# Choosing and fetching the first expert item during attention, in a fused attention, expert and feed-forward kernel

## The chip, the cores and the metric

The kernel runs as one program on one core of one Trainium2 chip. The metric is the device time of one execution in microseconds (us); lower is better. The engines are PE (TensorE, matmuls, with its weight loads shown as PEld), DVE (VectorE), ACT (ScalarE), POOL (GpSimd) and SP (SyncE, which here only issues DMAs).

## The reference

Three stages follow one another. All data is fp32.

```python
# 1 attention: q, k, v of shape (4, 12, 448, 64)
q_n, k_n = rmsnorm(q, g_q), rmsnorm(k, g_k)
attn = softmax(q_n @ k_n.T / 8);  x = attn @ v        # then (4*448, 768) tokens
# 2 experts: 8 experts, one per token
logits = normalize(x) @ normalize(expert_emb).T / tau
e = argmax(logits);  gate = softmax(logits)[e]
x = gate * (relu(x @ w1[e]) @ w2[e])                  # w1 768x1024, w2 1024x768
# 3 feed-forward: h = x @ w_in; out = max(0.01 * h, h) @ w_out   # 768x2048, 2048x768
```

## The kernel before

To keep fp32 accuracy every product is made of three matmuls on operands split in two parts: a rounded high part (type fp32r, made by ACT, `w1_hi`) and the rest (`w1_lo` = raw minus high, made by DVE, some of it by POOL).

**Attention** (`attention`, lines 15 to 483) goes over 48 heads (4 batches of 12), software-pipelined: iteration m of every engine's loop works on heads m-2 to m+2 at once, in an order written out by hand per engine. For the next head ACT squares q and k (L311), DVE sums (L394), POOL takes the power -0.5 (L159, L161), splits v (L147), scales and splits k (L177, L183, L187) and scales q (L193); PE transposes them (L229, L236), makes scores (L221, L222), transposes the probabilities (L244), multiplies by v (L258, L259) and by `mix` (L266), which folds the two halves of v's split and appends 8 expert logits of this head. DVE takes the row maxima (L401), splits the probabilities (L407) and stores the scaled result to `x_tok` (L421). POOL's order in an iteration is `split_k`, `norm_q`, `invert_rms`, `split_v`, `norm_k`, `norm_k_hi`, `guard_sums` (lines 197 to 211). SP loads the heads, writes x to `x_rows` in DRAM six heads late (L106), and between them loads the 14 chunks of expert 0's w1 and w2.

**Routing** (`routing`, lines 510 to 788) is a stage of its own behind a barrier of all engines. DVE sums the logits over heads, finds each token's expert (one-hot), counts, ranks within the expert, and makes of rank and expert a slot: an item (128 tokens of one expert, 21 items) and a lane. PE turns the table round (16 matmuls, L626) so that each slot knows its row of x (`slot_rows`). ACT squares x for the norms (L612) and DVE makes the gates.

**Experts** (`experts`, lines 791 to 1149): for item n POOL gathers 128 rows of x (L880), PE transposes them (L933), `product1` (L953 to L955, 6 chunks of 6 matmuls), relu on ACT (L1029), `transpose_h` (L964), `product2` (L983 to L985, 8 chunks of 6 matmuls), and POOL scatters the result (L886). SP loads an item's weights only where the expert is a new one; the split into high and low part is made again for every item. In the steady state `product2` of item n-1 stands between `product1` of items n and n+1, so that PE has work while item n+1 is split:

```python
    product1(n)
    transpose_x(n + 1, 1 - u)
    product2(n - 1, 1 - u, 0, C2 // 2)
    transpose_h(n, u)
    product2(n - 1, 1 - u, C2 // 2, C2)
```

**Feed-forward** (`feed_forward`, line 1152 on) gathers the rows by tiles, scales them by the gates and makes the two products.

The functions that the change touches:

## Time and profile before

| | |
|---|---|
| time, median of 3 runs (lowest, highest) | 1293.85 us (1293.66, 1295.03) |
| profiled execution: own time, its span | 1296.19 us, 1294.5 us |
| busy, share of the span: PE, DVE, ACT, POOL | 95%, 69%, 59%, 43% |
| mean granted clock of TensorE | 0.973 |
| attention, from the start to the last `x_tok` | 0 to 350.3 us |
| routing, then experts, to the last `product2` | 351.6 to 371.8, then to 776 us |
| DMA | 126.4 MB, mean 98 GB/s |

The span is the time from the first to the last instruction of the profiled execution. Its own time is 2.3 us above the median of the runs. An engine's busy share says how long it worked, not whether anything waited for it. A granted clock of 1.00 is 2.4 GHz, of 0.50 1.2 GHz.

### The profile page before, as it was taken

The page shows a single profiled execution, that of the slowest core. Times are in us where ns is not written, and L with a number is a line of the kernel's source. Part 1 is how long each engine was busy: PE and PEld are TensorE (multiplying, and loading weights), DVE is VectorE, ACT ScalarE, POOL GpSimd, SP SyncE. Part 2 cuts the span into 40 slices and gives each one's busy share as a digit, 9 for nine tenths or more (in the row PEclk, how much of TensorE's full clock was granted, in tenths as well). Part 3 has the DMA queues.
Part 4 walks back from the last instruction along what each step waited for, and adds up shares of the span by engine and source line. Part 5 has one row for each costly group of instructions (what it writes and reads, how often), then busy time and mean ns, then how long its engine had stood idle before and what let it go on. Part 6 is the DMA issues. An engine that isn't in the chain of part 4 may idle for free. (4 is left out here: it accounts for less than half of the span.)

```text
span 1294.5 us, 21003 instructions
## 1 busy us (share of the span) xinstructions
PE 1226.4 (95%) x6890; PEld 1097.1 (85%) x6890; DVE 894.2 (69%) x1257; ACT 757.6 (59%) x1434; POOL 553.3 (43%) x581
## 2 busy tenths in 40 slices
PE   5999999999748999999999995999999999999998
PEld 4888888888637988998899884999999999999997
DVE  4999999999757999999999973554432245552222
ACT  4999999999748777877787754222331122221111
POOL 6888888888335777667766740000000000000000
PEclk8999999999959999999999996999999999999999
DMA  1234333322103643664364014112232322211122
GB/s 50 75 103 116 97 105 93 83 67 72 29 28 120 244 142 128 244 244 147 124 242 147 38 49 122 49 49 62 74 92 62 91 65 74 70 44 49 56 86 73
DMA packets 99977, 126.42 MB, mean 98 GB/s; under 512 B 28568, under 2 KB 81048, under 8 KB 99872
## 3 DMA queue, kind: packets, MB, share of 16 engines
q1 hardware_dynamic: 92416, 103.07, 26.0%
q0 software_dynamic: 3360, 16.52, 3.5%
q10 hardware_dynamic: 4096, 5.51, 1.2%
q8 instruction: 57, 0.93, 0.3%
q14 instruction: 48, 0.39, 0.1%
HBM read 193.88 MB, written 19.27 MB: 165 GB/s over the span
## 5 line engine op out<-in xcount | busy, mean ns | idle before, releaser
L1010 ACT CAST w_hi<-w_raw 128x768 fp32r<-128x768 f32 (+1 forms) x294 | 249.7, 931 | 14.5 <-DMA w_raw<-moe_w_in 13.4
L1080 DVE TENSOR_TENSOR w_lo<-w_raw,w_hi 128x1024 fp32r<-128x1024 f32 x84 | 186.9, 2261 | 9.7 <-POOL w_lo L899 7.0
L1490 DVE TENSOR_TENSOR out_lo<-out_raw,out_hi 128x384 fp32r<-128x384 f32 x64 | 35.7, 558 | 169.5 <-ACT out_hi L1399 169.5
L1281 PE MATMUL ps_acc<-yT_hi,in_hi 128*128 128x448 f32 x384 | 142.9, 372 | 2.1 <-DVE yT_lo L1476 2.1
L899 POOL TENSOR_TENSOR w_lo<-w_raw,w_hi 128x1024 fp32r<-128x1024 f32 x42 | 105.8, 2520 | 91.3 <-ACT w_hi L1010 91.0
L1311 PE MATMUL ps_acc<-gT_hi,out_hi 128*128 128x448 f32 x384 | 142.6, 371 | 0.0
L1393 ACT ACTIVATE small_h<-ps_acc 128x448 f32<-128x448 f32 x64 | 34.9, 545 | 183.4 <-PE ps_acc L1283 183.4
L1282 PE MATMUL ps_acc<-yT_hi,in_lo 128*128 128x448 f32 x384 | 141.9, 370 | 0.0
L1283 PE MATMUL ps_acc<-yT_lo,in_hi 128*128 128x448 f32 x384 | 141.9, 369 | 0.0
L1313 PE MATMUL ps_acc<-gT_lo,out_hi 128*128 128x448 f32 x384 | 140.5, 366 | 0.0
L1312 PE MATMUL ps_acc<-gT_hi,out_lo 128*128 128x448 f32 x384 | 140.4, 366 | 0.0
L1399 ACT CAST out_hi<-out_raw 128x384 fp32r<-128x384 f32 x64 | 32.8, 513 | 179.9 <-PE ps_acc L1313 179.6
L1089 DVE TENSOR_TENSOR w_lo<-w_raw,w_hi 128x768 fp32r<-128x768 f32 x126 | 135.1, 1137 | 0.0
L407 DVE TENSOR_TENSOR pT_lo<-ps_pt,pT_hi 112x448 fp32r<-112x448 f32 x192 | 115.1, 620 | 27.6 <-ACT pT_hi L355 27.5
L346 ACT ACTIVATE probs<-ps_s,neg_max 112x448 f32<-112x448 f32 x192 | 122.7, 644 | 3.6 <-DVE neg_max L401 3.6
L1498 DVE TENSOR_TENSOR g_sb<-ps_acc,small_h 128x448 f32<-128x448 f32 x64 | 40.0, 625 | 116.3 <-ACT small_h L1393 116.3
L983 PE MATMUL ps_y<-w_hi,hT_hi 128*128 128x384 f32 x336 | 116.8, 348 | 1.5 <-issue 1.3
L893 POOL TENSOR_TENSOR w_lo<-w_raw,w_hi 128x768 fp32r<-128x768 f32 x42 | 105.7, 2518 | 22.9 <-ACT w_hi L1010 21.4
L401 DVE TENSOR_REDUCE neg_max<-ps_s 112x1 f32<-112x448 f32 x192 | 113.3, 610 | 2.0 <-PE ps_s L222 1.8
L984 PE MATMUL ps_y<-w_lo,hT_hi 128*128 128x384 f32 x336 | 113.5, 338 | 0.0
L985 PE MATMUL ps_y<-w_hi,hT_lo 128*128 128x384 f32 x336 | 113.5, 338 | 0.0
L953 PE MATMUL ps_h<-w_hi,xT_hi 128*128 128x512 f32 x252 | 101.3, 402 | 4.8 <-DVE w_lo L1080 2.9
(182 smaller groups left out, 2999.7 us busy)
## 6 DMA issues: line engine op xcount, KB each, us to landing
w_raw<-moe_w_in SPq DMA_DIRECT2D x84, 1536.0 KB
in_raw<-moe_w_in_in SPq DMA_DIRECT2D x32, 384.0 KB, 3.3
out_raw<-moe_w_out_in SPq DMA_DIRECT2D x64, 192.0 KB, 2.4
qk_raw<-q_in SPq DMA_DIRECT2D x48, 112.0 KB, 2.1
qk_raw<-k_in SPq DMA_DIRECT2D x48, 112.0 KB, 2.2
v_raw<-v_in SPq DMA_DIRECT2D x48, 112.0 KB, 2.0
x_rows<-x_tok SPq DMA_DIRECT2D x48, 112.0 KB, 2.5
out_rows<-o_sb ACTq DMA_DIRECT2D x26, 168.0 KB, 2.4
```

The costliest lines, as they stand in the source:

```text
L346: act.activation(probs[:, t, :], ps_s[0:R, t, 0:S], ACT.Exp, bias=neg_max[u][:, t:t + 1], accum_out=sums[u][:, t:t + 1]).then_inc(s_exp, 1)
L407: dve.tensor_tensor(pT_lo[u][:, :, cols], src, pT_hi[u][:, :, cols].bitcast(F32), ALU.subtract).then_inc(s_plo, 1)
L983: pe.matmul(out, hT_hi[u][:, c, :], w2_hi[:, c, cols], start=c == 0, stop=False)
L1010: act.copy(out[:, c, :], raw[:, c, :]).then_inc(s_hi, 1)
L1080: dve.tensor_tensor(w1_lo[:, c, :], w1_raw[:, c, :], w1_hi[:, c, :].bitcast(F32), ALU.subtract).then_inc(s_w1lo, 1)
L1089: dve.tensor_tensor(w2_lo[:, c, :], w2_raw[:, c, :], w2_hi[:, c, :].bitcast(F32), ALU.subtract).then_inc(s_w2lo, 1)
L1281: pe.matmul(h, in_hi[u][:, c, :], yT_hi[:, c, cols], start=c == 0, stop=False)
L1282: pe.matmul(h, in_lo[u][:, c, :], yT_hi[:, c, cols], start=False, stop=False)
L1283: last = pe.matmul(h, in_hi[u][:, c, :], yT_lo[:, c, cols], start=False, stop=c == C - 1)
L1311: pe.matmul(acc, out_hi[u][:, lhs], hi, start=first, stop=False)
L1312: pe.matmul(acc, out_lo[u][:, lhs], hi, start=False, stop=False)
L1313: last = pe.matmul(acc, out_hi[u][:, lhs], lo, start=False, stop=final)
```

## The change

The routing stage goes as a stage. What of it concerns the first three batches is done in attention, the rest at the head of the expert stage:

- POOL adds each head's 8 logits to a running sum (`add_logits`, in every iteration from 2 on), makes the index tables in iterations 4 to 7 (`tables`), the lane one-hots of the 12 early tiles in iterations 42 and 43 (`early_lanes`) and the gather of the first item's rows in iteration 45.
- DVE chooses the experts of three batches at the end of iteration 38, counts in 40, places in 41 and takes the expert with the most tokens as the first (`item_expert[0]`), turns the expert order in 42; PE has `early_ranks` (2 matmuls) and `first_rows` (12) before two of its `outputs`. SP loads the chosen expert's w1 and w2 behind the loads of heads 46 and 47.
- The first item's x is transposed and split at the end of attention (`transpose_first`, `x_hi_first`, `x_lo_first`).
- The expert stage begins with the last batch's choice on DVE, while ACT splits w1 high and POOL makes three chunks of `w1_lo`; PE's `place` (the table turned round) stands in the middle of `product1(0)`. Items 0 and 1 are of one expert and use one split; `product2(0)` is made before `product1(1)`.
- The squares of x for the gates are made from `x_rows`, one tile per item on ACT, and the gates at item 19 and 20.
- The rows of `x_rows` and `y_rows` are in the order of the output. `mix` holds 12 heads instead of 48, and the expert embeddings lie in `w1_raw`.

```diff
-    x_dest = x_rows.rearrange("(p t b) d -> p t (b d)", t=T, b=B)
+    x_dest = x_rows.rearrange("(b p t) d -> b p t d", p=R, t=T)
...
-        mix = sb("mix", [P, N, X])
+        mix = sb("mix", [P, H, X])
...
-                sp.dma_start(x_dest[:, :, bass.ds(n * D, D)], x_tok[:, :, bass.ds(n, 1), 0:D].rearrange("p t o d -> p t (o d)")).then_inc(s_x_out, 16)
+                sp.dma_start(x_dest[n // H, :, :, n % H * D:(n % H + 1) * D], x_tok[:, :, n, 0:D]).then_inc(
+                    s_x_early if n < EARLY else s_x_out, 16)
...
+            def first_weights(e, w, raw, C, s_in):
+                src = w[bass.ds(e, 1), :, :].rearrange("o (c p) n -> p (o c) n", p=P)
+                for k in range(2):
+                    chunks = slice(k * C // 2, (k + 1) * C // 2)
+                    sp.dma_start(raw[:, chunks, :], src[:, chunks, :]).then_inc(s_in[k], 16)
...
+                if n == N - 2:
+                    sp.wait_ge(s_pick, 1)
+                    e = sp.value_load(rt["item_expert"][0:1, 0:1], min_val=0, max_val=E - 1)
+                    first_weights(e, w1, w1_raw, C1, s_w1_in)
+                if n == N - 1:
+                    first_weights(e, w2, w2_raw, C2, s_w2_in)
...
+            def add_logits(n):
+
+                part = x_tok[:, :, n, D:X]
+                total = logits[:, n // H * T:(n // H + 1) * T, :]
+                pool.wait_ge(s_xc, n + 1)
+                if n % H == 0:
+                    pool.tensor_copy(total, part).then_inc(s_lg, 1)
+                else:
+                    pool.wait_ge(s_lg, n)
+                    pool.tensor_tensor(total, total, part, ALU.add).then_inc(s_lg, 1)
+            def early_lanes(m):
+
+                if m in (EARLY + 6, EARLY + 7):
+                    pool.wait_ge(s_lane, 1)
+                    pool.wait_ge(s_tables, 6)
+                    half = m - EARLY - 6
+                    for j in range(half * J0 // 2, (half + 1) * J0 // 2):
+                        last = pool.tensor_scalar(in_lane[:, j, :], rt["lane_index"][:, :], lane_f[:, j:j + 1], rt["row_plus"][:, j:j + 1],
+                                                  ALU.is_equal, ALU.mult)
+                    last.then_inc(s_in_lane, 1)
+                if m == EARLY + 9:
+                    pool.wait_ge(s_row_first, 1)
+                    pool.wait_ge(s_x_early, 16 * EARLY)
...
+                tables(m)
+                if m >= 2:
+                    add_logits(m - 2)
+                early_lanes(m)
+            add_logits(N - 2)
...
+                if n == EARLY + 2:
+                    early_ranks()
+                if n == EARLY + 7:
+                    first_rows()
...
+            def early_ranks():
+
+                pe.wait_ge(s_hot, 1)
+                some = hot[:, 0:J0, :].rearrange("p j e -> p (j e)")
+                pe.matmul(ps_tot, rt["ones"][:, :], some, start=True, stop=True)
+                pe.matmul(ps_rank, rt["before"][:, :], some, start=True, stop=True).then_inc(s_rank, 1)
+            def first_rows():
+
+                pe.wait_ge(s_in_lane, 2)
+                pe.wait_ge(s_in_first, 1)
+                for j in range(J0):
+                    last = pe.matmul(ps_row, in_lane[:, j, :], in_first[:, j, :], start=j == 0, stop=j == J0 - 1)
+                last.then_inc(s_first, 1)
+            def transpose_first():
+
+                pe.wait_ge(s_x_first, 16)
+                pe.wait_ge(s_exp, (N - 1) * T + 2)
+                for c in range(C1):
+                    last = pe.transpose(ps_s[:, c // 3, (c % 3) * P:(c % 3 + 1) * P], x_first[:, c * P:(c + 1) * P], ident[:, :])
+                last.then_inc(s_xt, 1)
...
+                if m == N - 1:
+                    transpose_first()
                 if m - 1 >= 0:
                     outputs(m - 1, (m - 1) % 2)
...
+                if n == EARLY + 2:
+                    early_totals()
+                if n == EARLY + 7:
+                    rows_of_first()
...
+            def early_choice():
+
+                dve.memset(scan[0][:, 0:8, :], 0.0).then_inc(s_step, 1)
+                dve.memset(scan[1][:, 0:8, :], 0.0).then_inc(s_step, 1)
+                dve.tensor_reduce(top[:, 0:J0], some, AX.X, ALU.max).then_inc(s_step, 1)
+                dve.tensor_tensor(is_top[:, :, :], some, top[:, 0:J0].unsqueeze(2).to_broadcast([R, J0, E]), ALU.is_equal).then_inc(s_step, 1)
+                dve.tensor_tensor(cand[:, :, :], is_top[:, :, :], e_index[:, :, :], ALU.mult).then_inc(s_step, 1)
+                dve.tensor_reduce(first_top[:, 0:J0], cand[:, :, :], AX.X, ALU.min).then_inc(s_step, 1)
+                dve.tensor_tensor(hot[:, 0:J0, :], e_index[:, :, :], first_top[:, 0:J0].unsqueeze(2).to_broadcast([R, J0, E]),
+                                  ALU.is_equal).then_inc(s_hot, 1)
+            def early_counts():
+                for k, hop in enumerate((1, 2, 4, 8)):
+                    a, b = scan[k % 2], scan[1 - k % 2]
+                    dve.tensor_tensor(b[:, 8:8 + J0, :], a[:, 8:8 + J0, :], a[:, 8 - hop:8 + J0 - hop, :], ALU.add).then_inc(s_step, 1)
+                dve.tensor_copy(rt["counts"][:, :], scan[0][:, 8 + J0 - 1, :]).then_inc(s_step, 1)
+                dve.tensor_tensor(ranks[:, :, :], ranks[:, :, :], scan[0][:, 8:8 + J0, :], ALU.add).then_inc(s_step, 1)
+                dve.tensor_tensor(ranks[:, :, :], ranks[:, :, :], hot[:, 0:J0, :].bitcast(F32), ALU.mult).then_inc(s_step, 1)
+                dve.tensor_reduce(rank_f[:, :], ranks[:, :, :], AX.X, ALU.add).then_inc(s_step, 1)
+            def early_places():
+                dve.tensor_copy(rank_i[:, :], rank_f[:, :]).then_inc(s_step, 1)
+                dve.tensor_scalar(lane_i[:, :], rank_i[:, :], P - 1, None, ALU.bitwise_and).then_inc(s_step, 1)
+                dve.tensor_scalar(blk_i[:, :], rank_i[:, :], 7, None, ALU.logical_shift_right).then_inc(s_step, 1)
+                dve.tensor_copy(blk_f[:, 0:J0], blk_i[:, :]).then_inc(s_step, 1)
+                dve.tensor_copy(lane_f[:, 0:J0], lane_i[:, :]).then_inc(s_lane, 1)
+                dve.tensor_reduce(most[:, :], rt["counts"][:, :], AX.X, ALU.max).then_inc(s_step, 1)
+                dve.scalar_tensor_tensor(most_e[:, :], rt["counts"][:, :], most[:, 0:1], e_index[:, 0, :], ALU.is_equal, ALU.mult).then_inc(s_step, 1)
+                dve.tensor_reduce(rt["chosen"][:, :], most_e[:, :], AX.X, ALU.min).then_inc(s_step, 1)
+                dve.tensor_scalar(rt["item_expert"][:, 0:1], rt["chosen"][0:1, :], float(E), None, ALU.add).then_inc(s_pick, 1)
+            def early_turn():
+                dve.tensor_scalar(turned[:, :], e_index[:, 0, :], rt["chosen"][:, 0:1], None, ALU.subtract).then_inc(s_step, 1)
+                dve.tensor_scalar(wrapped[:, :], turned[:, :], 0.0, float(E), ALU.is_lt, ALU.mult).then_inc(s_step, 1)
+                dve.tensor_tensor(turned[:, :], turned[:, :], wrapped[:, :], ALU.add).then_inc(s_step, 1)
+                dve.tensor_tensor(rt["ahead"][:, :, :], turned[:, :].unsqueeze(2).to_broadcast([R, E, E]),
+                                  turned[:, :].unsqueeze(1).to_broadcast([R, E, E]), ALU.is_gt).then_inc(s_step, 1)
+                dve.tensor_scalar(hit[:, :], first_top[:, 0:J0], rt["chosen"][:, 0:1], None, ALU.is_equal).then_inc(s_step, 1)
+                dve.wait_ge(s_step, 28)
+                dve.scalar_tensor_tensor(in_first[:, :, :], blk_f[:, 0:J0].unsqueeze(2).to_broadcast([R, J0, 2]), 0.0,
+                                         hit[:, :].unsqueeze(2).to_broadcast([R, J0, 2]), ALU.is_equal, ALU.mult).then_inc(s_in_first, 1)
+            def rows_of_first():
+
+                dve.wait_ge(s_first, 1)
+                dve.tensor_scalar(row_first[:, :], ps_row[:, 0:1], -1.0, None, ALU.add).then_inc(s_row_first, 1)
...
+            def last_logits():
+                total = logits[:, J0:J, :]
+                dve.tensor_tensor(total, total, x_tok[:, :, N - 1, D:X], ALU.add).then_inc(s_step, 1)
...
+                if m == EARLY + 2:
+                    early_choice()
+                if m == EARLY + 4:
+                    early_counts()
+                if m == EARLY + 5:
+                    early_places()
+                if m == EARLY + 6:
+                    early_turn()
+                if m == N:
+                    x_lo_first()
+            last_logits()
...
+    def splits(i):
+
+        return max(i - 1, 0)
+    def pool1(s):
+        return (0, 1, 2) if s == 0 else (1, 4)
+
+    def pool2(s):
+        return (1, 4, 6) if s == 0 else (1, 5)
...
-            load1(0)
-            load1(1)
-            load2(0)
-            for i in range(items - 2):
-                load1(i + 2)
+            load1(2)
+            for i in range(2, items):
+                if i + 1 < items:
+                    load1(i + 1)
+                load2(i)
+                if 2 <= i - 2 < J:
...
+            def lo1(i):
+                for c in pool1(splits(i)):
...
+            lo1(0)
             gather(1, 1)
-            for c in POOL1:
-                lo1(0, c)
+            gather(2, 0)
+            lo2(0)
...
+                if n >= 3:
+                    lo2(n - 1)
...
+                if n == items - 2:
+                    pool.wait_ge(s_xss, J)
+                    pool.tensor_tensor(x_norm[:, :], x_ss[:, :], consts["half"][0:R, 0:J], ALU.pow).then_inc(s_xnorm, 1)
...
+            def rank():
+                pe.wait_ge(s_hot, 1)
+                late = hot[:, J0:J, :]
+                pe.matmul(ps_tot, rt["ones"][:, :], late.rearrange("p j e -> p (j e)"), start=True, stop=True).then_inc(s_tot, 1)
+                pe.matmul(ps_rank, rt["before"][:, :], late.rearrange("p j e -> p (j e)"), start=True, stop=False)
+                for j in range(T):
+                    last = pe.matmul(ps_rank[:, j * E:T * E], rt["ones"][:, :], late[:, j:j + 1, :].to_broadcast([R, T - j, E]),
+                                     start=False, stop=j == T - 1)
+                last.then_inc(s_rank, 1)
+            def place():
+                pe.wait_ge(s_place, 1)
+                for j in range(J):
+                    if j >= J0:
+                        pe.wait_ge(s_place, j - J0 + 2)
+                    last = pe.matmul(ps_slot, in_lane[:, j, :], in_item[:, j, :], start=j == 0, stop=j == J - 1)
+                last.then_inc(s_put, 1)
...
-            transpose_x(0, 0)
+            rank()
+            product1(0, 0, C1 // 2)
+            place()
+            product1(0, C1 // 2, C1)
+            transpose_h(0, 0)
+            transpose_x(1, 1)
+            product2(0, 0, 0, C2)
...
+            def square_x(j):
+                act.wait_ge(s_chk[j % 2], uses(j, j % 2))
+                act.activation(x_chk[j % 2], x_chk[j % 2], ACT.Square, accum_out=x_ss[:, j:j + 1]).then_inc(s_xss, 1)
...
+                if 0 <= n - FIRST_CHK < J:
+                    square_x(n - FIRST_CHK)
...
+            for semaphore, count in stored:
+                act.wait_ge(semaphore, count)
+            for c in range(C2):
+                hi2(0, c)
+            relu(0, 0)
+            relu(0, 1)
+            h_hi(0, 0)
+            x_hi(1)
...
-            slot_column(0, 0)
+            late_choice()
+            block_starts()
+            late_places()
+            item_places()
+            rows_of_slots()
             slot_column(1, 1)
+            slot_column(2, 0)
             for c in range(C1):
-                if c not in POOL1:
-                    lo1(0, c)
-                if c == 2:
-                    x_lo(0)
+                lo1(0, c)
+            experts_of_items()
+            for c in range(C2 // 2):
+                lo2(0, c)
+            h_lo(0, 0)
+            x_lo(1)
+            for c in range(C2 // 2, C2):
+                lo2(0, c)
...
+                if n == items - 2:
+                    gate_exponents()
...
+            gates()
...
```

On POOL, in a head of the second batch. Before (L153 is `guard_sums`, L187 `split_k`):

```order
L177 TENSOR_TENSOR k_n<-qk_raw,rstd 112x256
L183 TENSOR_TENSOR k_hl<-qk_raw,rstd 112x4x64
L153 TENSOR_TENSOR sums_eps<-sums,eps_sum 112x4
L187 TENSOR_TENSOR k_hl<-k_n,k_hl 112x4x64
L193 TENSOR_TENSOR q_n<-qk_raw,rstd 112x4x64 x2
```

and now (L187 is `guard_sums`, L221 `split_k`):

```order
L211 TENSOR_TENSOR k_n<-qk_raw,rstd 112x256
L217 TENSOR_TENSOR k_hl<-qk_raw,rstd 112x4x64
L187 TENSOR_TENSOR sums_eps<-sums,eps_sum 112x4
L264 TENSOR_TENSOR logits<-logits,x_tok 112x32
L221 TENSOR_TENSOR k_hl<-k_n,k_hl 112x4x64
L227 TENSOR_TENSOR q_n<-qk_raw,rstd 112x4x64 x2
```

The addition of the logits has come between the two.

On DVE, at the end of attention's iteration 38. Before, the maxima of the next head (L401) are followed by the splits of this one (L407) and `x_tok`:

```order
L411 SCALAR_TENSOR_TENSOR qT_lo<-ps_tr,gain,qT_hi 128x448
L407 TENSOR_TENSOR pT_lo<-ps_pt,pT_hi 112x4x112
L401 TENSOR_REDUCE neg_max<-ps_s 112x1 x2
L407 TENSOR_TENSOR pT_lo<-ps_pt,pT_hi 112x4x112 x2
L421 TENSOR_TENSOR x_tok<-ps_ux,inv_sums 112x4x72
L401 TENSOR_REDUCE neg_max<-ps_s 112x1
```

and now, the seven instructions L590 to L602 of `early_choice` between L527 (maxima) and L533 (splits):

```order
L527 TENSOR_REDUCE neg_max<-ps_s 112x1 x2
L590 MEMSET scan 112x64
L591 MEMSET scan 112x64
L594 TENSOR_REDUCE top<-logits 112x12
L596 TENSOR_TENSOR is_top<-logits,top 112x96
L598 TENSOR_TENSOR cand<-is_top,e_index 112x96
L600 TENSOR_REDUCE first_top<-cand 112x12
L602 TENSOR_TENSOR hot<-e_index,first_top 112x96
L533 TENSOR_TENSOR pT_lo<-ps_pt,pT_hi 112x4x112 x2
L551 TENSOR_TENSOR x_tok<-ps_ux,inv_sums 112x4x72
```

`early_counts`, `early_places` and `early_turn` stand at the same place two, three and four iterations later.

On PE, at the head of the expert stage. Before:

```order
L933 MATMUL ps_xm<-ident,x_g 128x128 x6
L953 MATMUL ps_h<-w_hi,xT_hi 128x512
L954 MATMUL ps_h<-w_lo,xT_hi 128x512
L955 MATMUL ps_h<-w_hi,xT_lo 128x512
L953 MATMUL ps_h<-w_hi,xT_hi 128x512
L954 MATMUL ps_h<-w_lo,xT_hi 128x512
```

and now (L954 to L957 rank the last batch, L966 is `place`; 18 matmuls of `product1(0)` stand on either side of it):

```order
L954 MATMUL ps_y<-hot,ones 112x32
L955 MATMUL ps_y<-hot,before 112x32
L994 MATMUL ps_h<-w_hi,xT_hi 128x512
L995 MATMUL ps_h<-w_lo,xT_hi 128x512
L996 MATMUL ps_h<-w_hi,xT_lo 128x512
...
L966 MATMUL ps_y<-in_item,in_lane 128x22 x16
L994 MATMUL ps_h<-w_hi,xT_hi 128x512
L995 MATMUL ps_h<-w_lo,xT_hi 128x512
L996 MATMUL ps_h<-w_hi,xT_lo 128x512
```

The transposes of item 0 are gone from here, and the placing has come in.

## Rows read from the trace of the kernel before

**Rows 1.** Four stretches by engine: us, busy time (instructions), PE clock, DMA share, GB/s.

```profile
100.00:200.00 100.00, 99.66 (x715) 86.12 (x714) 91.48 (x178) 97.56 (x253) 84.96 (x134) 1.00 0.37 100
360.00:370.00 10.00, 3.63 (x16) 3.49 (x16) 8.65 (x31) 4.92 (x12) 3.32 (x1) 0.50 0.00 0
430.00:440.00 10.00, 10.00 (x56) 9.19 (x55) 10.00 (x10) 7.34 (x9) 6.67 (x3) 1.00 0.99 386
500.00:600.00 100.00, 100.00 (x542) 91.47 (x541) 100.00 (x83) 79.15 (x100) 68.27 (x32) 1.00 0.54 199
```

**Rows 2.** Timeline of one attention head: start, duration, engine, line, out<-in [idle before<-releaser].

```profile
251.25 1.15 DVE L407 TENSOR_TENSOR pT_lo<-ps_pt,pT_hi 112x448 fp32r<-112x448 f32 x2
251.36 0.73 POOL L187 TENSOR_TENSOR k_hl<-k_n,k_hl 112x256 fp32r<-112x256 f32 x1
252.03 0.17 PEld L222 LDWEIGHTS ps_s<-kT,qT_lo 128*112 128x112 f32 x1
252.23 0.53 PEld L229 LDWEIGHTS ps_tr<-ident,k_hl 112*128 112x128 f32 x4
254.12 0.20 POOL L159 TENSOR_TENSOR meansq<-sumsq,eps_d 112x8 f32<-112x8 f32 x1 [0.88 <-DVE sumsq L394]
255.50 0.41 ACT L323 CAST v_hl<-v_raw 112x256 fp32r<-112x256 f32 x1 [0.17 <-PE ps_ux L259]
255.99 0.73 POOL L147 TENSOR_TENSOR v_hl<-v_raw,v_hl 112x256 fp32r<-112x256 f32 x1
257.95 0.20 POOL L153 TENSOR_TENSOR sums_eps<-sums,eps_sum 112x4 f32<-112x4 f32 x1
```

**Rows 3.** Timeline of ACT: one copy per head, 41 heads apart.

```profile
61.63 0.53 ACT L317 COPY u_sb<-ps_ux 128x448 f32<-128x448 f32 x1
...
337.69 0.53 ACT L317 COPY u_sb<-ps_ux 128x448 f32<-128x448 f32 x1
```

**Rows 4.** Timeline: last store of attention, then relu of items 0, 1, 2 and 20.

```profile
349.88 0.46 DVE L421 TENSOR_TENSOR x_tok<-ps_ux,inv_sums 112x288 f32<-112x288 f32 x1 [3.53 <-PE ps_ux L266]
...
391.70 1.09 ACT L1029 ACTIVATE h_sb<-ps_h 128x512 f32<-128x512 f32 x2 [9.25 <-PE ps_h L955]
407.30 1.09 ACT L1029 ACTIVATE h_sb<-ps_h 128x512 f32<-128x512 f32 x2 [1.38 <-PE ps_h L955]
426.10 1.09 ACT L1029 ACTIVATE h_sb<-ps_h 128x512 f32<-128x512 f32 x2 [2.85 <-PE ps_h L955]
...
756.68 1.09 ACT L1029 ACTIVATE h_sb<-ps_h 128x512 f32<-128x512 f32 x2 [2.86 <-PE ps_h L955]
```

**Rows 5.** Timeline near the start of attention.

```profile
8.30 1.77 DVE L434 COPY mix<-fold 128x3072 f32<-128x3072 f32 x1
8.53 2.00 POOL L177 TENSOR_TENSOR k_n<-qk_raw,rstd 112x256 f32<-112x256 f32 x1
```

**Rows 6.** Timeline of POOL in routing: first and last of 11 table instructions.

```profile
351.57 0.19 POOL L586 MEMSET not_before<- 112x112 f32 x1 [7.44 <-POOLq L31]
...
353.48 0.15 POOL L602 IOTA free_row<- 128x21 f32 x1
```

**Rows 7.** Timeline of routing and the first gather.

```profile
354.89 0.29 DVE L646 TENSOR_TENSOR is_top<-logits,top 112x128 f32<-112x128 f32 x1
...
361.52 0.17 DVE L712 CAST slot_i<-slot_f 112x16 int32<-112x16 f32 x1
364.42 3.63 PE L626 MATMUL ps_slot<-in_item,in_lane 112*128 112x66 f32 x16 [6.95 <-DVE in_lane L733]
372.93 1.21 POOL L880 DMA_INDIRECT x_g<-x_rows,slot_in  x1 [4.61 <-DVE slot_in L1071]
```

**Rows 8.** Timeline in the expert stage: a DVE split beside POOL's, and one alone.

```profile
503.34 2.39 POOL L899 TENSOR_TENSOR w_lo<-w_raw,w_hi 128x1024 fp32r<-128x1024 f32 x1 [1.98 <-ACT w_hi L1010]
503.92 2.89 DVE L1080 TENSOR_TENSOR w_lo<-w_raw,w_hi 128x1024 fp32r<-128x1024 f32 x1
...
394.45 1.23 DVE L1080 TENSOR_TENSOR w_lo<-w_raw,w_hi 128x1024 fp32r<-128x1024 f32 x1
```

790 lines of the change are left out of this document (392 added, 398 removed).

## The prediction

> **What bounds the kernel now.** I read first the busy times of four stretches, to see which engine has room in which stage [rows 1]. In attention (the first row) PE works 99.7 of 100 us, ACT 97.6, DVE 91.5 and POOL 85: nothing is free there. In routing (the second) PE works 3.6 of 10 us, with a granted clock of 0.50, while DVE is busy with small operations. In the steady experts (the last) PE works all the time at clock 1.00, and item follows item without a gap; ACT works 79% of it.
>
> Then the timeline of one head [rows 2], to see who waits for whom at its shortest margin. `split_k` on POOL ends at 251.36 + 0.73 = 252.09, and PE loads it at 252.23 (L229): with about 0.06 for the semaphore, 0.08 us of slack. POOL's chain cannot start earlier, since `split_v` waits for ACT's rounding of v (255.50 + 0.41, then 255.99). On DVE the split L407 follows with no idle time before it, so what is put ahead of it comes late nearly whole. A head takes (337.69 - 61.63) / 41 = 6.73 us [rows 3].
>
> Last the way from attention to the first products [rows 4]: attention ends at 350.3, the routing stage starts at 351.6, the first relu of item 0 stands at 391.7 and that of item 2 at 426.1, 74.5 us behind 351.6. Of these, 41 us lie ahead of the first relu, and this is what the change attacks. From item 2 on, item follows item at (756.68 - 426.10) / 18 = 18.37 us, with ACT idle for 2.86 before each relu.
>
> The profiled execution took 1296.2 us itself, 2.3 above the median of 1293.85. I make the sum against 1296.2 and take 2.3 off at the end.
>
> **Attention, part by part.**
> A. `mix` is a quarter as large. Its copy took 1.77 us and a `k_n` beside it 2.00 [rows 5]. Gain 1.3 (bounds 0 and 2).
> B. `add_logits`, 46 times on POOL between `guard_sums` and `split_k`. Nothing in the trace has 224 elements; the nearest are 0.20 us for 4 and for 8 elements a partition and 0.73 for 256 [rows 2], which gives 0.20 + 28 x 2.1 ns = 0.26, about 0.20 of it as pitch. Less the 0.08 of slack, `transpose_k` comes 0.12 late in each head: 46 x 0.12 = +5.5. Bounds: 0 if PE or ACT can reorder their waits around it, +9 if nothing is absorbed.
> C. The tables took POOL 353.63 - 351.57 = 2.1 us [rows 6], and stand now in four heads: +2.1 (0 to 2.1).
> D. The early choice on DVE. A 96-element operation costs about 0.28 (0.29 for 128), a tiny one 0.17 to 0.21 [rows 7]. Choice 5 x 0.28 and two memsets, 1.7; totals 0.5; counts 2.2; places 9 x 0.2 = 1.8: +6.2. The turn, 1.3, lies beside POOL's lanes, which are longer. DVE operations also queue behind a running POOL operation: a 1024-element split took 2.89 beside POOL's and 1.23 alone [rows 8]. A POOL operation of attention takes 84.96 / 134 = 0.63 us and one runs 85% of the time [rows 1], so an operation that queues waits 0.85 x 0.32 = 0.27. Of the 21 or so here I take this for 6, those that read two SBUF tiles as the split does: +1.5 (0 to 5.5).
> E. Lane one-hots, 12 on POOL, 112 elements each in two heads. Between 0.20 and 0.73 [rows 2] I take 0.33 by the elements: +4.0 (3 to 5.5).
> F. PE: 14 matmuls, 0.23 each at half clock [rows 7], so about 0.12 at the full one: +1.7.
> G. The gather holds POOL 1.21 [rows 7] ahead of `transpose_k`: +1.3.
> H. Six more transposes at the end and the last heads' loads behind 3.1 MB of w1, which take 8 us at 386 GB/s [rows 1] where the loads have about a head and a half of lead: +0.8 (0 to 4).
> Sum: -1.3 + 5.5 + 2.1 + 6.2 + 1.5 + 4.0 + 1.7 + 1.3 + 0.8 = **+21.8**, bounds +12 and +29. Attention should end at about 372.
>
> **The start of the experts,** counted from the barrier. Both weights should be there: 6.3 MB take 16 us at 386 GB/s and are issued two and one heads before the end. POOL makes three chunks of `w1_lo` (2.4 to 2.8 each), until 9.1. Meanwhile DVE does the late choice, about 28 small operations up to the last batch's lanes, at the pitch of [rows 7]; I let three queue behind POOL's long ones. That leaves some 14 of them behind 9.1, and puts these lanes at 9.1 + 14 x 0.25 = 12.7, the slots, rows and two columns, which wait for the 16 matmuls of `place` (3.6 at half clock, [rows 7]), at 16.2; then DVE's three chunks of `w1_lo`, 1.23 each [rows 8], to 19.9. PE, which stood with clock 0.50 as in the second row of [rows 1], does the last chunk behind them, in all about 4 more by half clock for the first chunk and full for the rest. The first relu comes at 24.0. From there to the relu of item 1: the relu pair 1.1 [rows 4], eight transposes 0.9, rounding 1.1, split 1.2 with semaphores make 4.5, and then `product2(0)` and `product1(1)`, which together are an item less its 14 transposes, 18.4 - 1.6 = 16.8. From relu 1 to 2 nothing stands between but `product1`, as between 0 and 1 before: 407.30 - 391.70 = 15.6 [rows 4]. Item 2's relu stands at 24.0 + 21.3 + 15.6 = 60.9, against 74.5: **-13.6**. With the first relu at 18.5 (no queueing) it is -19, at 28 (POOL and DVE in series) -9.6. From item 2 on the order of products is the old one.
>
> **The end.** The gates, four DVE operations and POOL's power behind item 20, stand now before the feed-forward's first tiles: +0.6 (0 to 3). `square_x`, about 0.9 + 0.2 per item on ACT (a relu pair of 1024 elements takes 1.09), fits into its 2.86 of idle time: 0. If ACT's cover were gone it would cost 16 x 1 us.
>
> Net: 21.8 - 13.6 + 0.6 = **+8.8**: 1305.0 by this execution, 1302.6 by the median. In short, routing loses its 20 us of its own, but its operations come back where every engine is full, and the first item's cold start stays.
>
> **Rivals.**
> 1. Faster: idle times in a head take up the small work. For it speaks that POOL stands 0.88 idle before L159 and ACT 0.17 before L323 [rows 2], and DVE works only 91.5% [rows 1], 0.6 us a head. Then `add_logits`, tables and the queueing cost nothing (B, C, the 1.5 of D), and of the other inserts (6.2 + 4.0 + 1.7 + 1.3 + 0.8 = 14.0) a quarter vanishes. Attention -1.3 + 10.5 = +9.2, net 9.2 - 13.6 + 0.6 = -3.8: 1290.1. Against it: the idle time lies before L159, and the short margin before L229; POOL cannot work ahead of ACT's v. It decides by one point: whether L229 starts later. Chance 0.32.
> 2. All small operations queue. In the trace only large ones do, 2.89 beside 2.39 [rows 8], and 2.00 for the `k_n` of 256 elements beside a DVE copy [rows 5]. If the other 15 of D wait 0.27 each too, attention gets 4 more. Of the late choice only one operation then runs at each seam between POOL's, some 24 instead of 14 are left behind 9.1, and with their pitch of 0.25 the first relu comes 3 later: 8.8 + 7 = 15.8, 1309.6. Chance 0.18.
> The Trainium skill, SBUF — State Buffer, "Who interferes with whom", says that DVE and GpSimd share one pair of ports, which an instruction locks until it ends, and that this holds for a DVE instruction with two SBUF inputs or in a two-port mode. By that rule, the trace agrees for the large ones: DVE's split ends about when POOL's and then its own time have passed [rows 8]. It would put plain fp32 copies between SBUF tiles into the queue too, and by it the time is that of this rival; no row of before shows a small one blocked.
> 3. None of the small operations queues: -1.5 in D and the first relu at 18.5, -5.5 in the start. Net 8.8 - 1.5 - 5.5 = +1.8: 1295.7. Chance 0.12.
> 4. The change does not do what it says: the first weights or rows are late. At the 199 GB/s of the last row of [rows 1] the 6.3 MB need 32 us, where some 12 to 25 are to be had before the barrier. w1, which goes first, needs 16 of them; the gathered rows beside it then come 2 us late, and w2 is wanted only 20 us behind the barrier: +2, 1304.6. Chance 0.04.
>
> **How the numbers follow.** My forecast, 1302.6 with 1297 to 1309 as its own range, has 0.34. About 0.2%, 2.6 us, is what a measurement of this kernel can tell from no change, so 1291.3 to 1296.4 is the same. Faster takes rival 1 for the most part (0.29) and 0.03 of rival 3; same takes 0.03 of rival 1, 0.07 of rival 3 and 0.05 from the forecast's and rival 4's low end; the rest, 0.53, is slower. The range must reach from rival 1 with half of its own width below, 1285, to rival 2 with as much above, 1315.
>
> **What would show it.** In the profile of after: ACT's head period at 6.85 instead of 6.73 with L229's counterpart waiting for POOL's `split_k` (B); heads 38 to 45 longer by 12 to 15 us together (D to G); the last `x_tok` near 372; DVE's small operations no longer than 0.3 except beside POOL's splits (rivals 2 and 3); PE idle with clock 0.50 in the first 10 us of the experts; the first relu 24 and item 2's 61 us behind the barrier. I am wrong if the head period stays 6.73, which makes rival 1 the case; if the first relu comes beyond 28, which adds its delay whole; or if PE waits between items 2 and 20, where I cost everything at nothing.

## The result and the profile after

The changed kernel takes 1314.17 us (median of 4 runs, 1311.04 to 1319.03) against 1294.28 for the kernel before on the same chip: a ratio of 1.0157 with an interval of 1.0120 to 1.0194, 19.9 us slower. The forecast was 8.8 slower, the range reached to 1315. A second set of four runs gave 1312.19 and 1.0149 (1.0132 to 1.0167). The profiled execution took 1319.03 itself, span 1317.3, so it shows 22.8 us more than the span before, some 3 to 5 more than the medians do.

| stretch of the profiled execution | before | after | difference | forecast |
|---|---|---|---|---|
| attention, to the end of the last `x_tok` | 350.3 | 377.0 | +26.7 | +21.8 |
| from the next stage's start to item 2's relu | 74.5 | 62.5 | -12.0 | -13.6 |
| relu 2 to relu 20 | 330.6 | 332.8 | +2.2 | 0 |
| relu 20 to the feed-forward's first transpose | 30.9 | 38.0 | +7.1 | +0.6 |
| from there to the end of the span | 506.9 | 505.7 | -1.2 | 0 |

The stage's start is POOL's first table before, 351.6, and ACT's first rounding of w1 after, 378.3; both lie 1.2 us behind attention.

Stretches of after by engine (us; busy time and instructions of PE, PEld, DVE, ACT, POOL; PE clock, DMA share, GB/s), as in [rows 1]:

```profile
100.00:200.00 100.00, 99.71 (x714) 84.94 (x713) 91.14 (x179) 97.46 (x254) 88.39 (x150) 1.00 0.27 70
323.00:325.00 2.00, 0.00 (x0) 0.00 (x0) 2.00 (x6) 0.00 (x0) 2.00 (x3) 1.00 0.00 0
327.00:329.00 2.00, 2.00 (x10) 1.96 (x10) 0.00 (x0) 1.20 (x4) 1.92 (x4) 0.50 0.05 8
380.00:384.00 4.00, 2.84 (x10) 2.39 (x10) 3.93 (x3) 4.00 (x6) 4.00 (x2) 0.50 0.61 172
```

Attention in its middle is as full as it was. New are the second and third row: PE did nothing for 2 us in the middle of attention, and then ran with a granted clock of 0.50. The fourth row is the head of the experts.

ACT's copy of each head, as in [rows 3]:

```profile
136.54 0.53 ACT L436 COPY u_sb<-ps_ux 128x448 f32<-128x448 f32 x1
...
284.94 0.53 ACT L436 COPY u_sb<-ps_ux 128x448 f32<-128x448 f32 x1
...
334.13 0.54 ACT L436 COPY u_sb<-ps_ux 128x448 f32<-128x448 f32 x1
...
347.94 0.53 ACT L436 COPY u_sb<-ps_ux 128x448 f32<-128x448 f32 x1
...
364.19 0.53 ACT L436 COPY u_sb<-ps_ux 128x448 f32<-128x448 f32 x1
```

The first two copies are 22 heads apart: where only `add_logits` is inserted a head takes 6.745 us, against 6.735 before. The head before 334.13 took 14.4 and the next 13.8. Over heads 38 to 45, from 284.94 to 364.19, the trace has 25.4 us more than eight times 6.735, over heads 4 to 14 (the tables) 2.2.

What `add_logits` (L264) does in a head, as in [rows 2]:

```profile
252.43 0.25 POOL L264 TENSOR_TENSOR logits<-logits,x_tok 112x32 f32<-112x32 f32 x1
252.65 0.74 POOL L221 TENSOR_TENSOR k_hl<-k_n,k_hl 112x256 fp32r<-112x256 f32 x1
253.43 0.41 PEld L320 LDWEIGHTS ps_tr<-ident,k_hl 112*128 112x128 f32 x4 [0.16 <-POOL k_hl L221]
253.50 0.55 PE L320 MATMUL ps_tr<-ident,k_hl 112*128 112x112 f32 x4
255.73 0.68 ACT L456 ACTIVATE qT_hi<-ps_tr,gain 128x448 fp32r<-128x448 f32 x1
```

and before, beside [rows 2], ACT's copy of this head, the k transposes and the rounding of q:

```profile
250.13 0.53 ACT L317 COPY u_sb<-ps_ux 128x448 f32<-128x448 f32 x1
252.43 0.55 PE L229 MATMUL ps_tr<-ident,k_hl 112*128 112x112 f32 x4
254.65 0.68 ACT L337 ACTIVATE qT_hi<-ps_tr,gain 128x448 fp32r<-128x448 f32 x1
```

`split_k` (L221) now ends 2.18 behind the head's copy on ACT (251.21), and PE's weight load waits for it, 0.16. In [rows 2] the same load came 2.10 behind the copy (250.13), now it comes at 2.22: the 0.12 of the forecast. But the load stood 0.20 ahead of its matmul, and this lead takes the delay: the matmuls start 2.29 behind the copy, 2.30 before, and ACT rounds q 4.52 behind it in both. Over ten heads of each trace the medians say the same: load 2.09 before and 2.25 now, matmul 2.29 and 2.30. The delay ends on PE itself.

The head of iteration 42, with POOL's six lane one-hots:

```profile
321.31 4.69 POOL L273 TENSOR_SCALAR in_lane<-lane_index,lane_f,row_plus 112x128 fp32r<-112x128 f32 x6
326.75 1.01 PE L320 MATMUL ps_tr<-ident,k_hl 112*128 112x112 f32 x4 [4.61 <-POOL k_hl L221]
327.80 0.53 ACT L448 CAST kT<-ps_tr 128x448 fp32r<-128x448 f32 x1 [4.92 <-PE ps_tr L320]
```

One one-hot of 128 elements with two scalars from memory takes 4.69 / 6 = 0.78 us on POOL, more than the 0.73 of a subtraction of 256 elements [rows 2]. PE stands 4.61, and its four transposes then take 1.01 instead of 0.55. The clock stands at 0.50 for about 6.8 us in each of the two heads with the one-hots, and for about 3.4 in the one with the counts.

DVE in iterations 38 and 40: the operations that read two SBUF tiles while POOL works,

```profile
286.44 0.72 DVE L596 TENSOR_TENSOR is_top<-logits,top 112x96 f32<-112x96 f32 x1
287.19 0.55 DVE L598 TENSOR_TENSOR cand<-is_top,e_index 112x96 f32<-112x96 f32 x1
...
301.64 1.85 DVE L616 TENSOR_TENSOR scan<-scan 112x96 f32<-112x96 f32 x4
```

0.72, 0.55 and 4 x 0.46 instead of 0.25 to 0.29.

The head of the experts, POOL and DVE, then PE's `place` (L966) and DVE's chunks of `w1_lo`:

```profile
379.42 7.03 POOL L916 TENSOR_TENSOR w_lo<-w_raw,w_hi 128x1024 fp32r<-128x1024 f32 x3 [6.10 <-ACT w_hi L1057]
380.10 1.70 DVE L1148 SCALAR_TENSOR_TENSOR block_i<-totals,counts 112x8 int32<-112x8 f32 x1
381.83 2.31 DVE L1150 TENSOR_SCALAR block_i<-block_i 112x8 int32<-112x8 int32 x1
384.18 2.31 DVE L1152 CAST blocks<-block_i 112x8 f32<-112x8 int32 x1
386.52 0.22 DVE L1154 TENSOR_TENSOR passed<-ahead,blocks 112x64 f32<-112x64 f32 x1
...
389.64 2.36 PE L966 MATMUL ps_y<-in_item,in_lane 112*128 112x22 f32 x16 [0.71 <-DVE in_item L1184]
...
392.60 3.49 DVE L1248 TENSOR_TENSOR w_lo<-w_raw,w_hi 128x1024 fp32r<-128x1024 f32 x3
```

The three chunks of `w1_lo` on POOL take 7.03 us. Beside them an operation of 8 elements takes 1.70, the next two 2.31 each, though the last two read a single tile; the first one that starts when POOL is done takes 0.22. `place` ends at 392.0, 13.7 behind the start, and only then come DVE's chunks 3 to 5.

Behind them an operation of one partition meets POOL's splits of w2, and PE stands 3.83 before `product2(0)` for the low part of h, which stands behind it on DVE:

```profile
396.92 5.43 DVE L1209 TENSOR_SCALAR item_e<-item_e,chosen 1x21 f32<-1x21 f32 x1
...
406.88 0.41 PE L1024 MATMUL ps_y<-w_hi,hT_hi 128*128 128x384 f32 x1 [3.83 <-DVE hT_lo L1268]
```

The relu of items 0, 1, 2 and 20, as in [rows 4]:

```profile
400.16 1.09 ACT L1075 ACTIVATE h_sb<-ps_h 128x512 f32<-128x512 f32 x2 [10.21 <-PE ps_h L996]
...
425.25 1.08 ACT L1075 ACTIVATE h_sb<-ps_h 128x512 f32<-128x512 f32 x2 [21.10 <-PE ps_h L996]
...
440.77 1.09 ACT L1075 ACTIVATE h_sb<-ps_h 128x512 f32<-128x512 f32 x2 [7.14 <-PE ps_h L996]
...
773.56 1.08 ACT L1075 ACTIVATE h_sb<-ps_h 128x512 f32<-128x512 f32 x2 [2.63 <-PE ps_h L996]
```

Item 0's relu stands 21.9 behind the start, item 1's 25.1 behind that, item 2's 15.5 behind that.

The end of the experts: POOL's power, the first of the gates' operations on DVE, the exponent on ACT, and PE's idle time:

```profile
766.55 3.93 POOL L941 TENSOR_TENSOR x_norm<-x_ss,half 112x16 f32<-112x16 f32 x1
770.52 1.82 DVE L1221 TENSOR_SCALAR x_norm<-x_norm 112x16 f32<-112x16 f32 x1
774.60 0.31 ACT L1102 ACTIVATE exps<-shifted 112x128 f32<-112x128 f32 x1
776.51 0.47 PE L1024 MATMUL ps_y<-w_hi,hT_hi 128*128 128x384 f32 x1 [2.99 <-DVE w_lo L1256]
...
811.56 1.35 PE L1446 MATMUL ps_trf<-ident,y_g 112*128 112x112 f32 x6 [11.64 <-ACT y_g L1553]
```

The power holds POOL 3.93 us, DVE's next operation waits for POOL's splits again (1.82 for 16 elements), the exponent and with it ACT's next roundings wait for both, and PE stands 2.99 before `product2(19)`. Yet PE later stands 11.64 before L1446, where the gates could have been made for nothing.

### The profile page after: what moved, and what is told of

It is laid out like the page before. It is cut to its first block and busy times, and to the rows that moved or that the text cites. A ratio compares the mean times of both kernels' runs of the same rounds, so it can differ in the third digit from the quotient of the medians.

```text
span 1317.3 us, 21043 instructions
## 1 busy us (share of the span) xinstructions
PE 1237.8 (94%) x6906; PEld 1101.8 (84%) x6906; DVE 891.9 (68%) x1267; ACT 748.0 (57%) x1420; POOL 558.2 (42%) x638
## 3 DMA queue, kind: packets, MB, share of 16 engines
q1 hardware_dynamic: 94304, 108.58, 26.7%
## 5 line engine op out<-in xcount | busy, mean ns | idle before, releaser
L1057 ACT CAST w_hi<-w_raw 128x768 fp32r<-128x768 f32 (+1 forms) x280 | 238.8, 931 | 22.3 <-DMA w_raw<-moe_w_in 13.4
L1248 DVE TENSOR_TENSOR w_lo<-w_raw,w_hi 128x1024 fp32r<-128x1024 f32 x79 | 173.5, 2232 | 1.7 <-ACT w_hi L1057 1.6
L533 DVE TENSOR_TENSOR pT_lo<-ps_pt,pT_hi 112x448 fp32r<-112x448 f32 x192 | 115.1, 620 | 42.1 <-ACT pT_hi L474 41.9
L1256 DVE TENSOR_TENSOR w_lo<-w_raw,w_hi 128x768 fp32r<-128x768 f32 x119 | 132.3, 1174 | 1.2 <-ACT w_hi L1057 1.2
L527 DVE TENSOR_REDUCE neg_max<-ps_s 112x1 f32<-112x448 f32 x192 | 113.2, 610 | 2.1 <-PE ps_s L313 1.8
L994 PE MATMUL ps_h<-w_hi,xT_hi 128*128 128x512 f32 x252 | 101.5, 403 | 12.1 <-DVE w_lo L1248 10.2
L335 PE MATMUL ps_pt<-ident,probs 112*112 112x112 f32 x768 | 101.1, 265 | 7.1 <-DVE pT_lo L533 7.0
```

What stands on the lines that cost most here:

```text
L1057: act.copy(out[:, c, :], raw[:, c, :]).then_inc(s_hi, 1)
L1248: dve.tensor_tensor(w1_lo[:, c, :], w1_raw[:, c, :], w1_hi[:, c, :].bitcast(F32), ALU.subtract).then_inc(s_w1lo, 1)
L1256: dve.tensor_tensor(w2_lo[:, c, :], w2_raw[:, c, :], w2_hi[:, c, :].bitcast(F32), ALU.subtract).then_inc(s_w2lo, 1)
```

## The experiments

What each kernel shows by stage, from its profiled execution (att: what attention took; 4-14 and 38-45: us over the period of 6.735 in these heads; relu 0: from the stage's start; relu 1: from relu 0; 2-20: relu 2 to 20; end: relu 20 to the feed-forward). The sets a, b and c ran on three chips, on which the kernel before took 1293.97, 1294.88 and 1295.25 us in the median, so that a difference of a microsecond or two between sets says nothing:

| kernel | time, us | att | 4-14 | 38-45 | relu 0 | relu 1 | 2-20 | end |
|---|---|---|---|---|---|---|---|---|
| before | 1294.3 | 350.3 | 0 | 0 | 40.1 | 15.6 | 330.6 | 30.9 |
| changed, first set | 1314.2 | 377.0 | 2.2 | 25.4 | 21.9 | 25.1 | 332.8 | 38.0 |
| a0_again | 1312.2 | 377.0 | 2.3 | 26.3 | 21.3 | 25.4 | 325.7 | 37.8 |
| a1_lanes_dve | 1308.0 | 371.3 | 2.3 | 19.3 | 21.2 | 25.5 | 325.8 | 38.1 |
| a2_gates_end | 1305.5 | 374.9 | 2.2 | 25.4 | 21.9 | 25.1 | 327.5 | 30.7 |
| a3_start | 1311.8 | 375.6 | 2.3 | 23.5 | 15.5 | 27.9 | 329.0 | 37.8 |
| b1_start2 | 1308.6 | 377.3 | 2.3 | 25.4 | 15.1 | 21.6 | 327.4 | 37.2 |
| b2_spread | 1297.0 | 359.6 | 1.9 | 10.2 | 22.5 | 24.2 | 329.9 | 38.7 |
| b3_warm | 1311.0 | 370.6 | 2.6 | 19.0 | 21.1 | 25.6 | 327.6 | 36.6 |
| b4_all | 1280.9 | 361.9 | 2.0 | 9.8 | 15.4 | 21.4 | 329.8 | 30.9 |
| c1_all_again | 1279.5 | 359.1 | 1.9 | 9.9 | 15.4 | 21.6 | 325.7 | 30.7 |
| c2_two_adds | 1324.2 | 384.8 | 4.0 | 27.2 | 21.2 | 25.4 | 332.1 | 38.0 |
| c3_add_behind_q | 1282.2 | 357.6 | 0.2 | 9.3 | 15.1 | 23.1 | 325.9 | 30.8 |

**The changed kernel again.**

> The changed kernel once more, for a second trace and more times. If the delays of attention are fixed ones, the heads take the same times as in the first trace (14.4 and 13.8 us for the two with the lane one-hots on POOL, 10.8 for the one with the counts). The 8 us between its runs (1311 to 1319) I expect in the expert items, where some take 19.9 us and others 18.05: if it comes from there, another number of items is long this time. Time 1311 to 1319.

Attention repeats (377.0; 26.3 over in heads 38 to 45). Within it heads differ by up to 0.9: the one with the counts takes 11.7 for 10.8, the next 9.0 for 8.4, the first with one-hots 13.9 for 14.4. For the first of these the granted clock goes along: it stands at 0.50 for about 6.1 us here and 3.4 in the first trace. Relu 2 to 20 takes 325.7 instead of 332.8: in the first trace items 5, 7 and 9 took 19.9, here none does. That is 7 us, as much as the runs of this kernel scatter, and the place is the expected one. Why some items are long in one execution and not in the next stays open; in these three PE waits 1.2 us for a `w_lo` of DVE.

**The lane one-hots on DVE.** In POOL's iterations 42 and 43 the six operations go, and DVE makes them behind its own at the same iterations:

```diff
-                        last = pool.tensor_scalar(in_lane[:, j, :], rt["lane_index"][:, :], lane_f[:, j:j + 1], rt["row_plus"][:, j:j + 1],
+                        last = dve.tensor_scalar(in_lane[:, j, :], rt["lane_index"][:, :], lane_f[:, j:j + 1], rt["row_plus"][:, j:j + 1],
```

> The 12 early lane one-hots move from POOL to DVE, six at the end of iteration 42 and six in 43. Theory A (they cost 0.78 us each on POOL and stop the chain split_k, transposes, scores; on DVE 0.28 each): the two heads take 6.74 + 1.7 + 1.4 (the turn) and 6.74 + 1.7 instead of 14.4 and 13.8, so 11 us less, about 1303. Theory B (the two heads are long because the first expert's weights load beside them, not because of POOL): the two heads stay over 12 us, and the time falls by less than 4.

```profile
323.31 1.62 DVE L656 TENSOR_SCALAR in_lane<-lane_index,lane_f,row_plus 112x128 fp32r<-112x128 f32 x6
...
332.77 2.79 DVE L656 TENSOR_SCALAR in_lane<-lane_index,lane_f,row_plus 112x128 fp32r<-112x128 f32 x6
```

0.27 each for the first six. The two heads take 11.8 and 10.5 instead of 13.9 and 13.7 in a0_again, 5.4 less; the time falls by 4.2. The one-hots' place is part of the cost, but 11 was too much: DVE's six operations, behind six others, make their head 5.1 longer for 3.9 of work, and the second six take 2.79, queued behind POOL. PE now stands 2.75 and 1.75 in these heads, and its clock falls to 0.50 in both again. Theory B falls: SP issues the first expert's w1 at 335.95 in the first trace, behind the first of the two long heads, and in that head's gap nothing loads (the second of the rows by engine, 0 GB/s).

**The gates at the end.** POOL's power stands behind `store_y` of item 19, the exponent behind ACT's last rounding, DVE's gates behind its last split:

```diff
-                if n == items - 2:
-                    gate_exponents()
...
             for c in range(C2 // 2, C2):
                 lo2(items - 1, c)
+            gate_exponents()
+            gates()
```

> The power on POOL, the exponent on ACT and the gates on DVE stand behind the last splits instead of in items 19 and 20, where PE later stands idle 11.6 us anyway. Theory A (POOL's power of 3.9 us holds up its splits and DVE, and exp on ACT waits for them): from the relu of item 20 to the first transpose of the feed-forward 31 us as before the change instead of 38, time about 6 less, 1308. Theory B (the end is long for another reason, the loads or the order of the last scatters): 38 stays, and the time with it.

```profile
766.16 1.09 ACT L1074 ACTIVATE h_sb<-ps_h 128x512 f32<-128x512 f32 x2 [2.64 <-PE ps_h L995]
...
796.89 1.35 PE L1444 MATMUL ps_trf<-ident,y_g 112*128 112x112 f32 x6 [11.67 <-ACT y_g L1551]
```

30.7 instead of 38.0 from item 20's relu to the feed-forward, 7 us; the medians differ by 6.7. Theory A holds: the end is as short as before the change. Power, exponent and gates moved together, so their shares are not separated.

**DVE alone at the start.** POOL's three chunks of the first `w1_lo` go to DVE, which makes one behind each step of the choice:

```diff
-        return (0, 1, 2) if s == 0 else (1, 4)
+        return () if s == 0 else (1, 4)
...
             late_choice()
+            lo1(0, 0)
             block_starts()
+            lo1(0, 1)
             late_places()
+            lo1(0, 2)
             item_places()
+            lo1(0, 3)
+            lo1(0, 4)
```

> POOL makes no chunk of the first w1_lo; DVE makes all six, one after each step of the late choice; the experts of the items are found before w2 is split. Theory A (three small DVE operations waited 1.7, 2.3 and 2.3 us for POOL's splits, and PE stood 4 us for that): relu of item 0 at 18 us from the start of the stage instead of 22, and item 1's 23 behind it instead of 25; 4 to 6 us less, about 1309. Theory B (what bounds the start is PE at half clock and its own products, not DVE): item 0's relu stays at 21 or later.

DVE (L1150 and L1152 are the two that took 2.31; L1148, which took 1.70, takes 0.17 too), then the last two lines of the search for the items' experts, POOL's `w2_lo` and PE's `product2(0)`:

```profile
379.53 0.17 DVE L1150 TENSOR_SCALAR block_i<-block_i 112x8 int32<-112x8 int32 x1
379.74 0.17 DVE L1152 CAST blocks<-block_i 112x8 f32<-112x8 int32 x1
...
391.82 5.92 DVE L1215 CAST item_expert<-item_e 1x21 int32<-1x21 f32 x1
392.36 5.35 POOL L923 TENSOR_TENSOR w_lo<-w_raw,w_hi 128x768 fp32r<-128x768 f32 x3
...
401.66 0.66 PE L1024 MATMUL ps_y<-w_hi,hT_hi 128*128 128x384 f32 x1 [6.36 <-DVE hT_lo L1268]
```

With POOL idle the three take 0.17 each, and relu 0 comes at 15.5, 6.4 earlier and better than the 18 I expected, at the same clock of 0.50 for PE's first chunks. So the half clock of the first chunks did not bound the start, DVE's wait did. It also brought a second stretch at half clock: in the first trace PE's last three chunks start at 393.96, have the clock at 0.50 until 397.5 and take 6.2, here they start at 388.03 with 1.00 and take 4.4, 1.8 of the 6.4. (The chunks changed engine and place together; of the two, only the queueing is seen in the rows.) But 2.8 come back where I expected a gain of 2: a cast of 21 elements on a single partition takes 5.92, until the last of POOL's three splits, which follow one another without a gap, and PE stands 6.36 for the low part of h behind it. The cast is recorded as starting 0.54 before the first split, so that it met the splits running is not shown. The median falls by 0.4.

**The same without POOL's `w2_lo`.**

```diff
-        return (1, 4, 6) if s == 0 else (1, 5)
+        return () if s == 0 else (1, 5)
```

> As a3_start, and POOL makes none of the first w2_lo either. In a3 a cast of 21 elements on DVE took 5.92 us, as long as POOL's three splits of w2, and PE stood 6.4 us for the low part of h behind it. Theory A (each small DVE operation that meets a running POOL split waits for its end, and for those that follow at once): item 0's relu at 15.5 us from the first rounding of w1 as in a3, item 1's 21.5 behind it instead of 27.9 (25.1 before), together 10 us less than the changed kernel, about 1302. Theory B (PE's half clock and the splits of w2 by DVE alone, eight at 0.9, bound it): item 1's stays over 25 behind.

15.1 and 21.6, item 2's relu at 52.2 instead of 62.2: the 10 us are there to the digit. In the medians only 3.6 show, and the runs of this kernel scatter by 11 us (1304.3 to 1315.3); the stage, of one trace, is what this verdict rests on.

**Early work in three places of a head.** Tables one operation a head over heads 4 to 14; DVE's 42 early operations, lane one-hots among them, from one list, 1 or 2 before each of the splits `split_lo(m, 0)` and `split_lo(m, 1)`, which wait for ACT, and the rest at the end:

```diff
+                    slot(m, 'A')
                     split_lo(m, m % 2, 0)
...
+                    slot(m, 'B')
                     split_lo(m, m % 2, 1)
...
-                if m == EARLY + 2:
-                    early_choice()
+                slot(m, 'C')
```

> In attention: POOL's tables one operation a head over 11 heads; all early work of DVE, the 12 lane one-hots too, in three places of each head (one or two operations before each of the two splits that wait for ACT, the rest at the end) over heads 37 to 44. Theory A (a POOL operation of 0.2 us more per head stays hidden by ACT's squares; small DVE work is free before the splits that wait for ACT, 0.55 us a head; and no stall of PE is long enough to halve its clock): heads 4 to 14 at 6.75, heads 38 to 45 together 12 us over the period instead of 25, time about 14 less, 1298. Theory B (all of it is paid wherever it stands): heads 4 to 14 pay 2.4 us together as before, heads 38 to 45 over 18.

Heads 38 to 45 pay 10.2 instead of 25.4 (and 26.3): theory A, by more than expected. Two things are in this: the one-hots' move to DVE alone had brought 19.3 (a1), the rest is the spreading. Of the four heads with five or six operations two cost 0.8 and 1.3, two 0.2 each; what is left is 4.6 in the one with ten, and 1.5 and 1.3 in the last two, with the other eight one-hots and PE's rows. In the one with ten the clock stands at 0.50 for about 6.4 us; the same head takes 10.6 and 10.7 in b4_all and c1_all_again, with about 3.4 at 0.50, and 9.1 in c3_add_behind_q, where the clock stays 1.00. The tables pay 1.9 instead of 2.3: there theory B holds, an operation of 0.2 on POOL costs 0.17 a head once `add_logits` stands before it. The time falls by 15 to 17.

**Keeping the clock.**

```diff
             def transpose_k(n, u):
-                pe.wait_ge(s_khl, n + 1)
                 if n > 0:
                     pe.wait_ge(s_qlo, n)
+                if n in (EARLY + 8, EARLY + 9):
+                    for i in range(32):
+                        t = i % T
+                        pe.transpose(ps_tr[:, t * R:(t + 1) * R], ident[0:R, :], ident[0:R, 0:R])
+                pe.wait_ge(s_khl, n + 1)
```

> The changed kernel with the lane one-hots on POOL as they were, and 32 transposes of a constant on PE, written where the k transposes go, while PE waits for POOL in the two heads of the one-hots. Theory A (the two heads lose 7.4 us for 4.7 of POOL's work since the granted clock falls to 0.50 after 4 us of idle PE, and the rest of the head runs at half speed): the clock stays 1.00, the heads take 11.7 and 11.4 us instead of 14.2 and 13.8, time 4 to 5 less, about 1308. Theory B (the rest is POOL's own chain for q behind the one-hots): the heads stay as long, or longer by what the extra transposes cost.

POOL's one-hots, the added transposes and the k transposes that follow, then the stretch behind 325.51:

```profile
320.08 4.68 POOL L273 TENSOR_SCALAR in_lane<-lane_index,lane_f,row_plus 112x128 fp32r<-112x128 f32 x6
320.73 3.23 PE L321 MATMUL ps_tr<-ident 112*128 112x112 f32 x32
325.51 0.60 PE L324 MATMUL ps_tr<-ident,k_hl 112*128 112x112 f32 x4 [1.56 <-POOL k_hl L221]
```

```profile
326.00:328.00 2.00, 2.00 (x17) 1.87 (x15) 0.24 (x1) 1.84 (x5) 1.92 (x4) 1.00 0.14 39
```

POOL holds PE as long as before, 4.68, but the transposes take 0.60 instead of 1.01, the clock stays 1.00, and the two heads take 11.6 and 11.4 instead of 13.9 and 13.7, 4.7 less together, as theory A has it. Of the 14.8 us that the first trace shows for the two heads, 5 or so are the clock. (Attention is 6.4 shorter in all; 2.2 of it is the head with the counts, 9.4 here and 11.7 in a0_again, which the edit does not touch: here its clock stays 1.00 too. The same head takes 10.7 to 11.0 in the six traces where it stands at 0.50 for about 3.4 us. Why it did not fall here, no run shows.) The median shows 1.2 of it.

**All in one,** b1, b2 and a2 together, and once more.

> b1_start2, b2_spread and a2_gates_end in one. If the costs lie in three separate stages, they add: 10 + 14 + 7 less than the changed kernel's 1312, about 1281, which is below the kernel before. If they hide one another (the saved time of one stage comes back as a wait for weights in the next), it stays above 1290.

> b4_all once more, with more rounds, for its interval against the kernel before. If its 1280.9 us stands, 1277 to 1287 and a ratio under 0.995; if the first one was a lucky chip or run, above 1290.

The relu of item 2 of c1_all_again, whose first rounding of w1 stands at 360.36:

```profile
412.89 1.09 ACT L1091 ACTIVATE h_sb<-ps_h 128x512 f32<-128x512 f32 x2 [7.12 <-PE ps_h L1012]
```

1280.93, then 1279.51 with a ratio to the kernel before of 0.9875 (0.9854 to 0.9896). The stages add, and this version is 15.7 us faster than the kernel before, 33 faster than the change as made. Attention 359.1 (+8.8), item 2's relu at 52.5 (-22.0), the end 30.7.

**A second addition.** In every head, behind the first, with its result unused:

```diff
                     pool.tensor_tensor(total, total, part, ALU.add).then_inc(s_lg, 1)
+                pool.wait_ge(s_twice, n)
+                pool.tensor_tensor(unused[:, :, :], part, part, ALU.add).then_inc(s_twice, 1)
```

> The changed kernel with a second addition of the same size on POOL in every head, its result unused. The first cost 0.01 us a head although the k transposes came 0.12 later; the tables, one a head on top of it, cost 0.16 each. Theory A (behind the 0.08 us before the transposes lie some 0.15 more, in which ACT is still at its squares, and the first addition has used them up): the second is paid nearly whole, heads at 6.90 to 6.95 us, 7 to 9 us over the whole. Theory B (small POOL work is hidden by its 0.7 us of idle time in each head, and the tables cost something else): the heads stay at 6.75.

```profile
202.64 0.23 POOL L268 TENSOR_TENSOR unused<-x_tok 112x32 f32<-112x32 f32 x1
202.83 0.74 POOL L223 TENSOR_TENSOR k_hl<-k_n,k_hl 112x256 fp32r<-112x256 f32 x1
203.62 0.39 PEld L324 LDWEIGHTS ps_tr<-ident,k_hl 112*128 112x128 f32 x4 [0.34 <-POOL k_hl L223]
203.62 0.60 PE L324 MATMUL ps_tr<-ident,k_hl 112*128 112x112 f32 x4
205.86 0.64 ACT L460 ACTIVATE qT_hi<-ps_tr,gain 128x448 fp32r<-128x448 f32 x1
```

A head takes 6.90 us and attention 7.8 more than in a0_again; the median grows by 12.1, of which items 2 to 20 make another 6.4 in this trace. The load now waits 0.34 and comes 2.40 behind the head's copy (201.22). This is past the 2.30 at which the matmuls stood, so they come at 2.40 too, PE's work behind them 0.16 late, and ACT's rounding of q at 4.64 for 4.52. Theory A has the number right: the first 0.2 us were free, the second cost 0.155. It has the cover wrong: ACT rounds k 3.07 behind the copy in all three traces, before, after and here. What the first addition used up is the load's lead over its matmul, not ACT's squares.

**The addition behind `norm_q`.**

```diff
                     norm_q(m + 1, (m + 1) % 2)
+                if m >= 2:
+                    add_logits(m - 2)
                 if m + 2 < N:
                     invert_rms(m + 2, (m + 2) % 2)
```

> b4_all with the addition of the logits moved from before split_k to behind norm_q, where POOL then stands idle 0.7 us for the sums of squares. Theory A (what a small POOL operation costs is decided by its place: ahead of split_k it is paid, in that idle time not): heads 4 to 14, with one table operation each, at 6.75 instead of 6.92, 1.8 us less; the time 1 to 3 less than b4_all. Theory B (each us of POOL is paid once its 85% are exceeded, wherever it stands): heads 4 to 14 stay at 6.9 or the addition there delays the power and all heads grow.

Heads 4 to 14 pay 0.2 instead of 1.9, so the place decides: with the lead used up, what stands ahead of `split_k` is paid, what stands in the idle time before the power is not. The k load is back at 2.09 behind the copy. In the times the 1 to 3 us less that I expected do not show (1282.2 against 1280.9 and 1279.5). In the traces attention is 1.5 shorter than in c1_all_again, but relu 1 comes 1.5 later; PE's clock stands at 0.50 in 380 to 382 there, where it is 1.00 in c1_all_again. Whether the edit brings this is open.

## Why the prediction was right, and where it was not

The direction held, and so did the shape: attention pays more than the start of the experts gives back. The range held by 0.8 us, with luck: its upper end was set by rival 2's width, and 1314.2 is nearer to rival 2's 1309.6 than to the forecast. The medians are 11 us above the forecast, the traces 14.0: attention 4.9, the start 1.6, items 2 to 20 2.2 and the end 6.5 too low, less 1.2 behind it. Attention comes that near by luck too: B was 5.2 too high and hid half of the 10.8 by which E was too low.

- **A, C, F, G** held. The tables cost 2.2 (2.1). The first head comes 1.4 earlier (1.3), though this varies by 2 us from execution to execution. The heads with PE's rows and the gather cost 1.3 and 1.5 (3.0 together). Of H's 0.8 the trace shows 0.2 behind the gather's head.
- **B fell.** The operation was priced right (0.25 for 0.26; it has 32 elements a partition, the 224 of the text is a slip). I took the start of the k transposes' weight load for the point that decides, and forecast 5.5. The load starts 0.12 later, as worked out, and it costs 0.01 a head, since the load runs 0.20 ahead of its matmul and the matmul starts as before. The step that failed was to take the load's slack, 0.08, for PE's. c2 shows that the cover was 0.05 us from its end: the argument was right for the second operation, not for the first. The head period stayed 6.74, which I had named as the sign that rival 1 is the case. It is so for B alone: the tables, which rival 1 had at nothing, cost 2.2, and of the other inserts no quarter vanished.
- **D held in its sum, not in its path.** The operations took 2.1, 0.3, 3.0 and 1.9 us (forecast 1.7, 0.5, 2.2, 1.8, and 1.5 for the queue, together 7.7; measured 7.3). The heads grew by 1.9, 0.2, 4.0 and 1.7, 7.8 together, the one with the counts by 4.0 to 4.9: behind 3 us of DVE in one piece PE stands 1.96, its clock falls to 0.50, and the head's rest is slow. With the clock at 1.00 (b3) it grew by 2.7. Queueing hit the operations with two SBUF inputs and a few casts, as the forecast had it.
- **E was the largest miss.** I took 0.33 us an operation; B's own line gives 0.46 for 128 elements, and 0.78 is measured: an operation with scalars from memory is another kind than a subtraction, and no row of before had one on POOL. 12 x 0.78 = 9.4 instead of 4.0; the range I gave, 3.0 to 5.5, was bounded by operations of another kind. The rest of the 14.8 is the clock (5.3 against b3, 4.7 from a0_again), a term that the sum did not have. The turn lies beside the one-hots, as forecast.
- **The start** came out at 62.5 for 60.9. Three small operations queued, as forecast, and relu 0 was 2 earlier; relu 1 came 3.8 later behind it, for a tiny operation on item experts queues 5.43 behind POOL's `w2_lo`, a place where I let nothing queue.
- **Rival 2** (all small operations queue) is half true. At the start single-input operations wait as well. In attention most with a single input do not: 0.15 to 0.17 while POOL runs, one cast 0.59. The Trainium skill, SBUF — State Buffer, "Who interferes with whom", lets a one-input operation outside the two-port modes pass, and names cast and `tensor_scalar` among the forms that can enter such a mode and are then locked out. The 2.31 of the cast and of the 8-element shift fit the second half, the 0.16 and 0.17 of the 12-element ones the first; which mode each ran in no run here shows.
- **The end** was forecast at 0.6 and cost 7.1. I placed the gates' operations behind item 20, while the kernel has them in items 19 and 20. I costed the four DVE operations and the power, but not who stands behind them: POOL's own splits, ACT's roundings behind the exponent, and `product2(19)`. a2 gives all of it back: behind the last splits the forecast place costs nothing.
- **The steady items**, forecast 0: 18.1 us where none is long, 18.37 before, and up to 19.9 in some. So items 2 to 20 give 4.9 back in a0_again (325.7 for 330.6) and cost 2.2 in the first trace, where PE waits in four of them, which was a sign of being wrong. Why the short ones are 0.28 shorter than before, no run tests. The squares fit into ACT's idle time (2.63 before the relu of item 20).

## What to carry to other kernels

Follow a delay past its first waiter to the work that sets the period (here the load was late and its matmul was not), and price an inserted operation by its place: here the same 0.2 us on POOL cost nothing as the first, 0.16 as the second, and nothing again behind `norm_q`. In a dense stage put small work in ones and twos before waits that are there anyway, not in one block that leaves TensorE idle, and keep chains of small VectorE operations off stretches in which GpSimd runs long ones back to back. Work that nothing waits for yet, as the gates, belongs into the largest idle time ahead of its consumer.

## What the runs showed of the hardware

- TensorE stood idle 4.6 us in the middle of attention, from a granted clock of 1.00 (2.4 GHz), and came back at 0.50 (1.2 GHz) for about 6 us. Behind shorter stalls it went either way: 1.96 us in the head with the counts was followed by 0.50 (3.4 us in the first trace, 6.1 in a0_again), 1.50 in c1_all_again too, but 1.90 in b3 and 1.73 in c3 were not. With transposes of a constant in the gap of the one-hots the clock stayed 1.00 (b3), for 2.3 us a head.
- A weight load of TensorE that came 0.16 us later (2.25 instead of 2.09 behind ACT's copy) cost nothing, since it had run 0.20 ahead of its matmul; at 2.41 it held up the matmul and with it the head, by 0.155.
- A small VectorE operation beside GpSimd splits can wait for one of them (2.31 us each for two operations of 8 elements beside splits of 2.34) or for all that follow without a gap: 5.92 us for a cast of 21 elements on one partition, beside three splits that together took 5.35. With no split running (a3_start and b1_start2) the same three take 0.17 each.
- A GpSimd one-hot of 112 x 128 with two scalars from memory takes 0.78 us, on VectorE 0.27.
